# Third and fourth unit of w2 in one transfer of 32768 bytes a row, issued behind the first two experts' first layers

## What is computed

```python
kv = einsum('bhsd,bhse->bhde', k, v)             # q, k, v: 8 x 8 x 576 x 64
out = einsum('bhsd,bhde->bhse', q, kv)
attn = out / sqrt(mean(out * out, -1) + 1e-6) * g_norm
x = attn as 4608 rows of 512                      # (batch, token) x (head, dim)
logits = x @ phi                                  # phi: 512 x 32, 8 experts with 4 slots each
slot_input = softmax_over_rows(logits).T @ x      # 32 slots x 512
for e in range(8):
    h = maximum(slot_input[e] @ w1[e], 0)         # w1[e]: 512 x 1024
    slot_out[e] = h @ w2[e]                       # w2[e]: 1024 x 512
result = softmax_over_slots(logits) @ slot_out    # 4608 x 512
```

## Time and profile before

| | |
|---|---|
| median of 3 runs | 171.92 us (171.84 to 171.95) |
| profiled execution, its own time | 171.83 us |
| its span (first to last recorded instruction) | 170.5 us |
| matmuls busy (PE) | 149.9 us, 88% of the span |
| ScalarE, VectorE, GpSimd busy | 52%, 51%, 35% |
| moved by DMA | 71.65 MB, 420 GB/s in the mean |
| granted TensorE clock | 0.97 of 2.4 GHz in the mean |

### The profile page before, as it was taken

The page is one execution under the profiler, slowest core; times in us unless marked ns, Lnnn a source line. Parts: engine busy times, 40 slices in busy tenths (PEclk is TensorE's granted clock), DMA queues, the critical chain, the costliest instruction groups (busy, mean ns, idle before and its releaser), DMA issues.

```text
span 170.5 us, 4242 instructions
## 1 busy us (share of the span) xinstructions
PE 149.9 (88%) x1836; PEld 104.4 (61%) x1836; DVE 86.8 (51%) x185; ACT 89.1 (52%) x230; POOL 59.7 (35%) x73
## 2 busy tenths in 40 slices
PE   7988897989999899999899998989999989989200
PEld 3467776979678888896697674346655533554000
DVE  1122156283677266762946698823888136318300
ACT  3036576796975986859759864202233044418300
POOL 7000707648357745377382679500000004000000
PEclk9999999999999999999999999999999999999755
DMA  5999999999999999989999999999999999999996
GB/s 184 420 423 432 426 430 429 482 416 435 484 410 408 458 428 415 434 384 467 400 465 392 459 409 407 450 429 415 430 427 446 452 434 392 414 422 443 411 455 288
DMA packets 4365, 71.65 MB, mean 420 GB/s; under 512 B 790, under 2 KB 790, under 8 KB 922
## 3 DMA queue, kind: packets, MB, share of 16 engines
q1 hardware_dynamic: 3994, 71.18, 97.9%
q0 software_dynamic: 352, 0.20, 0.4%
HBM read 61.94 MB, written 9.44 MB: 419 GB/s over the span
## 4 chain that ended last, share of the span: by engine, by line
PE 59%; DMA 13%; ACT 12%; DVE 6%; SPq 2%; issue 1%
PE psum L215 59%; DMA arena<-in_kv_dram 13%; ACT bd L215 3%; ACT sq L215 3%; ACT xall L215 2%; SPq L215 2%; DVE logits L215 1%; DVE ms L215 1%; ACT part L215 1%; ACT arena L215 1%; ACT d L215 1%; DVE part L215 1%; ACT r L215 1%; DVE acc L215 1%; DVE r L215 0%
## 5 line engine op out<-in xcount | busy, mean ns | idle before, releaser
L215 PE MATMUL psum<-bd,arena 128*128 128x192 f32 (+1 forms) x320 | 56.1, 335 | 2.0 <-ACT bd L215 1.6
L215 PEld LDWEIGHTS psum<-bd,arena 128*128 128x128 f32 (+1 forms) x320 | 45.4, 179 | 8.7 <-ACT bd L215 2.9
L215 DVE TENSOR_REDUCE ms<-sq 128x16 f32<-128x1024 f32 (+1 forms) x19 | 22.1, 1162 | 32.5 <-ACT sq L215 32.2
L215 POOL TENSOR_TENSOR part<-part,r 128x512 f32<-128x512 f32 x17 | 17.8, 1049 | 49.5 <-DVE r L215 49.5
L215 POOL TENSOR_TENSOR xall<-xall,r 128x512 f32<-128x512 f32 x34 | 34.8, 1043 | 0.0
L215 ACT ACTIVATE sq<-psum 128x512 f32<-128x512 f32 x36 | 21.5, 598 | 12.3 <-PE psum L215 12.1
L215 PEld LDWEIGHTS psum<-arena 128*64 128x64 f32 (+1 forms) x640 | 19.0, 137 | 8.1 <-DMA arena<-in_kv_dram 3.3
L215 PE MATMUL psum<-arena 128*64 128x64 f32 (+1 forms) x640 | 21.7, 226 | 2.1 <-DMA arena<-in_kv_dram 2.0
L215 ACT COPY xall<-psum 128x512 f32<-128x512 f32 x34 | 20.6, 606 | 0.0
L215 ACT COPY part<-psum 128x256 f32<-128x256 f32 (+1 forms) x38 | 13.6, 359 | 8.8 <-DVE part L215 7.6
L215 DVE TENSOR_REDUCE logits<-part 128x64 f32<-128x512 f32 (+1 forms) x18 | 17.9, 992 | 0.0
(11 more groups left out here) (80 smaller groups left out, 126.8 us busy)
## 6 DMA issues: line engine op xcount, KB each, us to landing
arena<-in_w_dram SPq DMA_DIRECT2D x4, 4096.0 KB, 23.5
arena<-in_w_dram SPq DMA_DIRECT2D x4, 2048.0 KB, 20.0
arena<-in_t_dram SPq DMA_DIRECT2D x1, 6912.0 KB, 36.0
arena<-in_w_dram SPq DMA_DIRECT2D x2, 3072.0 KB, 22.7
arena<-in_kv_dram SPq DMA_DIRECT2D x2, 2304.0 KB, 23.4
arena<-in_kv_dram SPq DMA_DIRECT2D x1, 4608.0 KB, 42.6
arena<-in_kv_dram SPq DMA_DIRECT2D x1, 3584.0 KB, 32.2
arena<-in_kv_dram SPq DMA_DIRECT2D x3, 1152.0 KB, 13.4
```

The costliest lines, as they stand in the source:

```text
L215: inst = getattr(engine, method)(*args, **kwargs)
```

## The change

Units 3 and 4 of w2 become one entry of `W_ROWS`, so one transfer of 128 rows of 32768 bytes (4096 KB) in place of two of 2048 KB. The host lays the two units side by side for it. The transfer is issued behind `expert_h(1)`, since it overwrites the places of both ("w1", 0) and ("w1", 1). Both places in `arena` stay what they were (72 and 88 are neighbours).

```diff
@@ -45,8 +45,7 @@
     (("w1", 5, None),),
     (("w2", 2, 0), ("w1", 6, None)),
     (("w1", 7, None),),
-    (("w2", 3, None),),
-    (("w2", 4, None),),
+    (("w2", 3, None), ("w2", 4, None)),
     (("w2", 5, None), ("w2", 6, None)),
     (("w2", 7, None),),
 )
@@ -984,9 +983,8 @@
 
     step_over(steps.pop())
     expert_h(0)
+    expert_h(1)
     load_w("w2", 3)
-    expert_h(1)
-    load_w("w2", 4)
     expert_y(0, 0)
     combine(0)
     expert_h(2)
```

## The result

The changed kernel took 172.78 us in the median of the first comparison, where the kernel before took 171.92: a ratio of 1.0047, with a 95% interval from 1.0034 to 1.0059. So it is slower, by 0.5 to 0.9 us. One of the five executions in the first comparison, the profiled one, ran at a mean granted clock of 0.56 and took 244 us; it is left out of the ratio and its profile is not used. All rows of "after" here are from the first experiment, the same kernel, whose profiled execution took 172.45 us with a span of 171.1.

What follows compares the result with a forecast made beforehand. The DMA queue was taken as the bound: profiled execution 171.83 us, less 0.05 for the queue, plus 0 for the slip, gave 171.78; the median lies 0.09 above, so 171.9 us, range 171.6 to 172.8.

Steps and rivals of the forecast that it cites:

- The DMA queue is the bound, and a transfer issued at 117.7 comes in time: Merged w2 transfer, issued at 117.72 us in place of 116.00: hidden by the full queue, some 6 us of cover.
- One transfer less, and longer rows, are worth 0.05 us: Units 3 and 4 in the DMA queue: price between -0.1 and +0.1 us, taken as a gain of 0.05 us.
- The fixed cost of about 2.0 us for each DMA: Faster rival, fewer transfers pay more: by the skill's figure 169.9 us; chance 0.05 of a gain over 0.34 us.
- TensorE waits for both units and slips by 1.7 us, and nothing behind makes it up: At `expert_y(4, 0)`: waits from 133.0 us for the arrival at 134.8; every store 1.7 us later, the last at 161.3.
- The clock falls in the pause: Slower rival: TensorE idle some 1.7 us before 134.9, clock falls to 1.2 GHz; 173.3 us, or 175.1; chance 0.16.
- The last store has a slack of 2.1 us: Last store (3072 KB): can be issued 2.1 us later without cost, bounds 1.0 and 2.6, so the 1.7 us slip fits.
- The first stores of half 0 are issued long before the weights have landed: Early stores of the result's half 0: claimed to be issued long before the weights land; no size given.
- The sum's term for the slip: TensorE's slip of 1.7 us, hidden by the last store's slack, adds 0 to the forecast time.
- the slip is more than the slack: Slower rival at the last store: with slack of only 1.0 us the end moves by 0.7 us, to 172.6; chance 0.11.
- the stated range: Forecast range for the time, 171.6 to 172.8 us, near enough to 8 in 10; leaves out the clock rival.
- Only the slowest DMA engine sets the end, so the others' dry time costs nothing: At the end of the last store: argument against the slack rival, that engines ending earlier cost 0.

Runs made afterwards that it cites:

- the first experiment: The changed kernel run once more, nothing else changed, for a profile at full clock, against the kernel before: 172.39 us against 171.84, ratio 1.0030.

## Why the prediction was wrong

*The DMA queue is the bound, and a transfer issued at 117.7 comes in time:* right. It landed at 134.8, as foretold, and the last weights at 149.4 as before.

*One transfer less, and longer rows, are worth 0.05 us:* nothing speaks against it, and no run can tell 0.05 us. The kernel with unit 4 first, in two transfers, and the merged one differ by 0.04 us in the median, within their spread. The fixed cost of about 2.0 us for each DMA that the Trainium skill gives (DMA: Bandwidth & Descriptors, the anatomy of one DMA) did not come back as time here.

*TensorE waits for both units and slips by 1.7 us, and nothing behind makes it up:* right in mechanism and nearly in size. 1.91 us of idle time, 1.8 us of slip, last store issued at 161.44 (161.3 foretold).

*The clock falls in the pause:* it did not; and nine matmuls in the place of the pause lost as much.

*The last store has a slack of 2.1 us:* the last two stores were 1.5 us late in one run and cost nothing that can be told, so their slack is at least 1.5, within the bounds of 1.0 and 2.6. The 1.8 us of the changed kernel were not tried alone, but there the last two landings stay 7.2 us apart.

*"The first stores of half 0 are issued long before the weights have landed":* this is the step that failed. I dismissed them in a sentence without a row, by the landing of the last weights at 149.4. That landing is the last of 16 engines; the stores are cut so finely, it seems, because the engines do not end together (146.4 to 149.3 us). The stretch that loses starts at 146, when the first of the 16 is done. The small stores of SP and GpSimd were issued from 140.15 to 143.7 before and from 141.95 to 145.5 after; all still ahead of 146, and yet too late: four of their packets took 1.7 to 3.6 times as long as others of their size. The sum's term for the slip was 0; it measured 0.5 to 0.6 us in one comparison and 0.8 to 0.9 in the other. My rival "the slip is more than the slack" named the right kind of cause and nearly the right price (0.7 us), but at the last store, where it is not. That 172.39 and, barely, 172.78 lie inside the stated range is luck: its upper part was there for that rival.

*Only the slowest DMA engine sets the end, so the others' dry time costs nothing:* this argument against that rival is unsafe. The long packets start between 146.6 and 148.2 us, before the last engine has done its weights (149.4), and those of SP, which stand in the queue behind the weights, so fell on engines that were not the slowest then. The 0.5 us are found again in every later landing. Time lost by an early engine can make it the slowest. That it did so here is argued from the three late steps of the last landing; the records do not name a packet's engine.

What stays open: why a packet takes longer when its store is issued 1.8 us later. The share of the DMA engines does not fall where the rate does, since the long packets count as busy. Why the two queues' stores cost so much more together than one by one was not settled. No version was found that beats the kernel before: leaving out the fills or cutting the last store gave nothing back.

## What to carry to other kernels

A merged transfer arrives as a whole: whoever read its first half waits for the second. That price stands even where the transfer itself costs nothing, and it is read from the matmuls' own schedule (here 1.8 us), before the bytes. Where DMA is the bound, ask for each store behind the wait, not only the last, when the first of the DMA engines runs out of older work (here 146.4 us); the landing of a whole transfer (149.4) tells only when the last one does.

## What the runs showed of the hardware that was not expected

The DMA share of a stretch can stay at 0.96 to 1.00 while its rate falls from 418 to 394 or 355 GB/s; in a DMA-bound stage the rate is the number to compare, and behind it the durations of packets of one size (here 234 ns and, in the hand-over, up to 1018 ns for 6144 bytes). Issuing the last small store of half 0 (384 KB) took SP 0.59 us at 143.68 and 0.96 us at 145.48, 0.60 to 2.35 us in the other runs where it was late; why is not shown. And TensorE's clock stayed at 2.4 GHz through 1.91 idle us between two runs of 64 matmuls. Behind the last matmul of the kernel before it stood at 1.2 GHz after 1.1 idle us, behind the last one of the changed kernel only after 4.2 us (last matmul ended at 160.78, fall at 164.96). The length of a pause alone did not decide it here.
